# A fused three-stage kernel on one core: the fifth pass of the up projection as two 64-row matmuls, chunks in pairs

## The reference

```python
# x: (2, 4096, 192); weight: 8 heads x 7 taps, each head has 24 of the 192 channels
out = np.einsum('hk,bskhg->bshg', w, x_unf)          # a causal mix of 7 tokens, w = softmax(weight)
h = x @ w_in                                          # 8192 x 192 @ 192 x 2048
g = np.where(h >= 1, h, np.where(h <= -1, 0.0, (h + 1) ** 2 / 4))
x = g @ w_out                                         # 8192 x 2048 @ 2048 x 192
h = x @ w_in2
r = np.maximum(h, 0.0)
g = s * (r * r) + b
return g @ w_out2
```

## Time and profile before

| what | value |
|---|---|
| median of 3 runs | 1198.95 us |
| span of the profiled execution (first to last instruction) | 1196.3 us |
| PE busy | 1177.9 us, 98% of the span, 5138 matmuls |
| PEld busy | 963.1 us, 81%, 5138 loads |
| DVE busy | 934.8 us, 78% |
| ACT busy | 614.1 us, 51% |
| DMA | 20.31 MB, mean 17 GB/s |

### The profile page before, as it was taken

How to read it: one execution, slowest core, us unless ns; L and a number is a source line. 1 busy time by engine, 2 the same in 40 slices (tenths; PEclk the granted TensorE clock), 3 DMA queues, 4 the chain that set the end, 5 groups by cost and what they waited for, 6 DMA issues and landing times.

```text
span 1196.3 us, 14126 instructions
## 1 busy us (share of the span) xinstructions
PE 1177.9 (98%) x5138; PEld 963.1 (81%) x5138; DVE 934.8 (78%) x842; ACT 614.1 (51%) x619; POOL 3.4 (0%) x16
## 2 busy tenths in 40 slices
PE   6999999999999999999999999999999999999998
PEld 3787888888888888888888888888888888888886
DVE  8999987778786877868778687787787878765555
ACT  5446654555545554545545554555545455454544
POOL 1000000000000000000000000000000000000000
PEclk9999999999999999999999999999999999999999
DMA  6003100000000000000000000001000000000000
GB/s 176 1 1 97 53 1 1 27 27 1 0 0 27 26 0 0 0 27 26 0 0 0 27 26 0 0 0 53 0 0 0 0 26 0 0 1 1 27 0 27
DMA packets 12360, 20.31 MB, mean 17 GB/s; under 512 B 1072, under 2 KB 5168, under 8 KB 12336
## 3 DMA queue, kind: packets, MB, share of 16 engines
q1 hardware_dynamic: 12256, 19.99, 5.9%
q0 software_dynamic: 64, 0.00, 0.0%
q10 hardware_dynamic: 16, 0.00, 0.0%
HBM read 13.70 MB, written 6.29 MB: 17 GB/s over the span
## 4 chain that ended last, share of the span: by engine, by line
PE 93%; DVE 5%; issue 1%; DMA 0%; SPq 0%; ACT 0%; DVEq 0%; ACTq 0%
PE h L653 46%; PE acc L666 28%; PE acc_rem L675 19%; DVE g L437 1%; DVE g_lo L455 1%; DVE mixed L489 1%; DVE mixed L503 0%; DVE mixed_rem L503 0%; DMA xraw_rem<-in_x 0%; DVE x_rem L516 0%; DVE up_lo L536 0%; DVE up_rem_lo L536 0%; DVE dn_lo L536 0%; DVE g L445 0%; DVE dn_rem L536 0%
## 5 line engine op out<-in xcount | busy, mean ns | idle before, releaser
L439 DVE SCALAR_TENSOR_TENSOR g<-r,scale,h 128x1024 f32<-128x1024 f32 x128 | 163.9, 1280 | 155.2 <-ACT r L287 154.4
L285 ACT ACTIVATE r<-h,half 128x1024 f32<-128x1024 f32 x128 | 143.1, 1118 | 272.0 <-PE h L653 264.8
L287 ACT ACTIVATE r<-h 128x1024 f32<-128x1024 f32 x128 | 131.7, 1029 | 284.9 <-PE h L653 284.3
L437 DVE TENSOR_TENSOR g<-h,r 128x1024 f32<-128x1024 f32 x128 | 156.6, 1223 | 93.3 <-ACT r L285 92.7
L458 DVE SCALAR_TENSOR_TENSOR g_lo<-g,shift,g_hi 128x1024 fp32r<-128x1024 f32 x128 | 163.7, 1279 | 0.0
L666 PE MATMUL acc<-g_hi,dn_hi 128*128 128x512 f32 x512 | 160.0, 394 | 3.1 <-DVE g_lo L455 1.6
L653 PE MATMUL h<-x_hi,up_hi 128*128 128x512 f32 x512 | 157.9, 390 | 3.0 <-DVE g L437 1.7
L653 PE MATMUL h<-x_rem,up_rem_hi 128*128 128x512 f32 x512 | 157.9, 390 | 2.5 <-DVE x_rem L516 2.5
L675 PE MATMUL acc_rem<-g_lo,dn_rem 128*128 128x512 f32 x512 | 157.9, 389 | 0.0
L675 PE MATMUL acc_rem<-g_hi,dn_rem 128*128 128x512 f32 x512 | 157.9, 389 | 0.0
L666 PE MATMUL acc<-g_lo,dn_hi 128*128 128x512 f32 x512 | 157.9, 390 | 0.0
(11 more groups left out here) (87 smaller groups left out, 963.3 us busy)
## 6 DMA issues: line engine op xcount, KB each, us to landing
xraw<-in_x SPq DMA_DIRECT2D x7, 518.0 KB, 4.4
out<-res SPq DMA_DIRECT2D x7, 512.0 KB, 3.3
stage<-in_moe_w_out SPq DMA_DIRECT2D x6, 384.0 KB, 3.4
xraw_rem<-in_x SPq DMA_DIRECT2D x14, 129.5 KB, 4.0
out<-res_rem SPq DMA_DIRECT2D x7, 256.0 KB, 3.6
stage<-in_moe_w_in SPq DMA_DIRECT2D x2, 512.0 KB, 5.2
stage<-in_moe_w_in SPq DMA_DIRECT2D x4, 256.0 KB, 5.2
xraw<-in_x SPq DMA_DIRECT2D x1, 512.0 KB, 4.2
```

Source lines behind the costliest of these rows:

```text
L285: nc.scalar.activation(r[k][:], h[k][:], ACT.Relu, scale=0.5, bias=half[:, 0:1]).then_inc(r_ready, 1)
L287: nc.scalar.activation(r[k][:], h[k][:], ACT.Relu).then_inc(r_ready, 1)
L437: nc.vector.tensor_tensor(g[k][:], h[k][:], r[k][:], ALU.max).then_inc(h_used, 1)
L439: nc.vector.scalar_tensor_tensor(g[k][:], r[k][:], scale[:, 0:1], h[k][:], ALU.mult, ALU.mult).then_inc(h_used, 1)
```

## The change

The fifth pass is made of 64-row matmuls: batch 0 uses rows 0 to 63 of the array and batch 1 rows 64 to 127 (`up_halves`), each reading only the half of `x_rem` with the high part. The product of the low weights with the low data, which the 128-row form added in, is no longer computed. For this the output of layer 0 must have its high half at rows 64t as the mixed data do: `y_rem` becomes its own tile of 128 x 512, and the ACT and DVE steps that write and split it become two of 64 x 512 each, where they were one of 64 x 1024.

`up` is replaced by `up_pair`: four full passes of chunk j, its two halves, the two halves of chunk j+1, and then the four full passes of chunk j+1. After it come down(j-2) and down(j-1). ACT and DVE follow: the rounding and the low part of chunk j-1 for even j now stand ahead of relu(j) and first(j). In DVE's layer 0 the second step of an odd chunk stands behind the low part of the even one, as before.

```diff
@@ -82,7 +82,7 @@
         mixed_rem = sb("mixed_rem", [P, T])
         shared = sb("shared", [P, B, T])
         fold = shared[0:REM]
-        y_rem = shared[REM:P]
+        y_rem = sb("y_rem", [P, T])
         y = sb("y", [P, B, T])
         res = sb("res", [P, B, T])
         res_rem = sb("res_rem", [REM, B, T])
@@ -141,6 +141,7 @@
         acc_drained = sem("acc_drained")
         fold_ready = sem("fold_ready")
         rem_drained = sem("rem_drained")
+        y_rem_ready = sem("y_rem_ready")
         main_summed = sem("main_summed")
         rem_summed = sem("rem_summed")
         half_drained = sem("half_drained")
@@ -337,11 +338,13 @@
                     act.wait_ge(h_ready, S_free + 1)
                 nc.scalar.activation(dst[0][:], y[:], ACT.Copy).then_inc(x_hi_done[1], 1)
 
-            def round_y_rem(phase, dst, S_free):
-                act.wait_ge(rem_drained, phase + 1)
-                if S_free is not None:
-                    act.wait_ge(h_ready, S_free + 1)
-                nc.scalar.activation(dst[2][REM:P], y_rem, ACT.Copy).then_inc(x_rem_hi_done[1], 1)
+            def round_y_rem(blk, dst, S_free):
+                for t in range(B):
+                    act.wait_ge(y_rem_ready, 2 * blk + t + 1)
+                    if S_free is not None:
+                        act.wait_ge(h_ready, S_free + 1)
+                    rows = slice(t * REM, (t + 1) * REM)
+                    nc.scalar.activation(dst[2][rows, t, :], y_rem[rows], ACT.Copy).then_inc(x_rem_hi_done[1], 1)
 
             def weights_hi(layer, n):
                 kind, q = PIECES[n]
@@ -356,14 +359,16 @@
 
 
                 for j in range(CH):
+                    if j == 0:
+                        if before is not None:
+                            round_g(before, S0 - 1, 1, G0)
+                    elif j % 2 == 0:
+                        round_g(layer, S0 + j - 1, (j - 1) % 2, G0 + j)
                     relu(layer, S0 + j, j % 2)
                     if j == CH - 1:
                         for f in last or ():
                             f()
-                    if j == 0:
-                        if before is not None:
-                            round_g(before, S0 - 1, 1, G0)
-                    else:
+                    if j % 2:
                         round_g(layer, S0 + j - 1, (j - 1) % 2, G0 + j)
                     if j == 1 and before is not None:
                         drain(before, S0, P0 - 1, blk_before)
@@ -407,12 +412,12 @@
                     12: [lambda: round_mixed(c + 2, X1, S0 - 1)]})
                 phase(0, 1, S1, P1, (c + 2) * CH, blk_before=c, extras={
                     4: [lambda: round_y(P0 - 1, X2, S1 - 1)],
-                    8: [lambda: round_y_rem(P0 - 1, X2, S1 - 1)]})
+                    8: [lambda: round_y_rem(c + 1, X2, S1 - 1)]})
 
             S0, P0 = (LOOPS + 1) * 2 * CH, (LOOPS + 1) * 2
             phase(1, 0, S0, P0, NB * CH, blk_before=NB - 1, extras={
                 4: [lambda: round_y(P0 - 1, X1, S0 - 1)],
-                8: [lambda: round_y_rem(P0 - 1, X1, S0 - 1)]})
+                8: [lambda: round_y_rem(NB - 1, X1, S0 - 1)]})
             phase(1, 1, S0 + CH, P0 + 1, NB * CH, blk_before=NB - 2)
             round_g(1, S0 + 2 * CH - 1, 1, None)
 
@@ -463,12 +468,17 @@
                 dve.wait_ge(fold_ready, phase + 1)
                 if layer == 0:
                     if not (isinstance(blk, int) and blk == 0):
-                        dve.wait_ge(x_rem_lo_done[1], blk)
-                    dst = y_rem
+                        dve.wait_ge(x_rem_lo_done[1], 2 * blk)
+                    nc.vector.tensor_tensor(y_rem[0:REM], acc_rem[0:REM, 0, :], fold[:, 0, :],
+                                            ALU.add).then_inc(y_rem_ready, 1)
+                    dve.wait_ge(y_rem_ready, 2 * blk + 1)
+                    nc.vector.tensor_tensor(y_rem[REM:P], acc_rem[0:REM, 1, :], fold[:, 1, :],
+                                            ALU.add).then_inc(y_rem_ready, 1)
+                    dve.wait_ge(y_rem_ready, 2 * blk + 2)
+                    dve.sem_inc(rem_drained, 1)
                 else:
                     dve.wait_ge(stored, 32 * (blk + 1))
-                    dst = res_rem[:]
-                nc.vector.tensor_tensor(dst, acc_rem[0:REM], fold, ALU.add).then_inc(rem_drained, 1)
+                    nc.vector.tensor_tensor(res_rem[:], acc_rem[0:REM], fold, ALU.add).then_inc(rem_drained, 1)
 
             def mix(blk, part, k):
 
@@ -523,9 +533,11 @@
                                         ALU.subtract).then_inc(x_lo_done[1], 1)
 
             def low_y_rem(blk, dst):
-                dve.wait_ge(x_rem_hi_done[1], blk + 1)
-                nc.vector.tensor_tensor(dst[2][0:REM], y_rem, dst[2][REM:P].bitcast(F32),
-                                        ALU.subtract).then_inc(x_rem_lo_done[1], 1)
+                for t in range(B):
+                    dve.wait_ge(x_rem_hi_done[1], 2 * blk + t + 1)
+                    rows, other = slice(t * REM, (t + 1) * REM), slice((1 - t) * REM, (2 - t) * REM)
+                    nc.vector.tensor_tensor(dst[2][other, t, :], y_rem[rows], dst[2][rows, t, :].bitcast(F32),
+                                            ALU.subtract).then_inc(x_rem_lo_done[1], 1)
 
             def weights_lo(layer, n):
 
@@ -539,18 +551,21 @@
             def phase(layer, before, S0, P0, blk_before=None, extras=None, last=None):
 
                 for j in range(CH):
+                    if j == 0:
+                        if before is not None:
+                            low(before, S0 - 1, 1)
+                    elif j % 2 == 0:
+                        low(layer, S0 + j - 1, 1)
                     first(layer, S0 + j, j % 2)
                     if j == CH - 1:
                         for f in last or ():
                             f()
-                    if j > 0:
-                        low(layer, S0 + j - 1, (j - 1) % 2)
-                    elif before is not None:
-                        low(before, S0 - 1, 1)
+                    if j % 2:
+                        low(layer, S0 + j - 1, 0)
+                    if layer == 0:
+                        second(S0 + j, j % 2)
                     if j == 1 and before is not None:
                         drain_rem(before, P0 - 1, blk_before)
-                    if layer == 0:
-                        second(S0 + j, j % 2)
                     for f in (extras or {}).get(j, ()):
                         f()
 
@@ -636,23 +651,41 @@
 
         @block.tensor
         def _(pe):
-            def up(layer, j, S, xs, split=None):
-
-
-                if not (isinstance(S, int) and S < 2):
-                    pe.wait_ge(h_used, S - 1)
+            def up_wide(layer, j, xs, start, split=None):
+
                 cols = slice(j * P, (j + 1) * P)
                 hi, lo, rem = xs
                 passes = [(up_hi[layer], hi, "hi"), (up_lo[layer], hi, None), (up_hi[layer], lo, "lo"),
-                          (up_rem_hi[layer], rem, "rem"), (up_rem_lo[layer], rem, None)]
+                          (up_rem_hi[layer], rem, "rem")]
                 for n, (w, v, part) in enumerate(passes):
                     if split and part:
                         for done, count in split[part]:
                             pe.wait_ge(done, count)
                     for t in range(B):
                         last = nc.tensor.matmul(h[j % 2][:, t, :], w[:, cols], v[:, t, :],
-                                                start=(n == 0), stop=(n == len(passes) - 1))
-                last.then_inc(h_ready, 1)
+                                                start=(start and n == 0), stop=(not start and n == 3))
+                return last
+
+            def up_halves(layer, j, xs, start):
+
+                cols = slice(j * P, (j + 1) * P)
+                for t in range(B):
+                    rows = slice(t * REM, (t + 1) * REM)
+                    last = nc.tensor.matmul(h[j % 2][:, t, :], up_rem_lo[layer][rows, cols], xs[2][rows, t, :],
+                                            start=start, stop=not start)
+                return last
+
+            def up_pair(layer, j, S, xs, split=None):
+
+
+                if not (isinstance(S, int) and S < 2):
+                    pe.wait_ge(h_used, S - 1)
+                up_wide(layer, j, xs, True, split)
+                up_halves(layer, j, xs, False).then_inc(h_ready, 1)
+                if not (isinstance(S, int) and S < 2):
+                    pe.wait_ge(h_used, S)
+                up_halves(layer, j + 1, xs, True)
+                up_wide(layer, j + 1, xs, False).then_inc(h_ready, 1)
 
             def down(layer, j, S, P0, final=False):
 
@@ -681,14 +714,15 @@
 
             def phase(layer, before, S0, P0, xs, split, weights=None):
 
-                for j in range(CH):
+                for j in range(0, CH, 2):
                     if weights and j in weights:
                         pe.wait_ge(w1_lo_done, weights[j])
```

(13 more changed lines are left out.)

## The result

The changed kernel takes 1191.69 us (median of 4 runs, 1191.32 to 1195.77), the kernel before 1199.09 (4 runs). The ratio is 0.9946 with a 95% interval of 0.9931 to 0.9961: 0.5% faster, 7.4 us by the medians. 1183.5 had been forecast, with 15.6 us of gain.

What follows compares the result with a forecast made beforehand. PE's matmul steps were taken to bound the kernel. From the 1196.3 us span, - 13.9 - 3.4 + 2.8 - 1.0 gave 1180.8, and 1183.5 us with the 2.65 us between span and median; range 1150 to 1222.

Steps and rivals of the forecast that it cites:

- group of halves: PE's fifth pass per pair: four halves with two division changes take 0.798 us in place of 0.907, -13.9 us for 128.
- drained sums: Each phase's first down no longer stops for ACT's copy of the sums: 13 x 0.26 = -3.4 us.
- start: Phase 0: DVE has 7.3 us more than PE, two downs hide 4.5, so PE loses +2.8 us.
- end: Last chunks: two downs cover the relu, round, low chain; the 1.46 us stop shrinks to about 0.5, -1.0 us.
- The bound: PE's matmul steps of 0.227 us set the time, one for one, until DVE becomes late.
- The halves: Four 64-row matmuls take 0.454 + 0.112 = 0.566 us, the second half starting one load behind the first.
- The changes: Each change of the array's division costs PE the restart alone, 0.116 us, between bounds of 0 and 0.28.
- emptying: Rival: at each change PE waits 0.16 us for the last matmul, then pays the 0.116 restart; 1211 to 1225 us, chance 0.20.
- Drain and overlap: By the skill's pages, halves start some 4 ns apart and each change drains 0.16 us: group 0.454 + 0.32 = 0.78 us.
- the drain case: Rival: drain but no restart at each change, group 0.78 to 0.89, 1181 to 1195 us; upper part, 1190 to 1199, chance 0.15.
- The rest rows: Splitting DVE's and ACT's rest-row steps adds 2.4 us on DVE and some 0.2 us a block on ACT, beside PE: nothing.
- DVE's cover: Layer 0 loop phases: DVE waits 8.8 us a phase for ACT's rounding, but 68.1 us fits in PE's 71.7: costs nothing.

Runs made afterwards that it cites:

- e2: Order of before on all engines, with the two 64-row halves in each chunk, so 512 division changes in place of 256: 1245.29 us, ratio 1.0388 to the kernel before.
- e3: Changed kernel with each half matmul issued twice, eight halves between the two changes of a pair: 1250.11 us, ratio 1.0427 to the kernel before.
- e4: Changed kernel with both batches' halves on rows 0 to 63 of the array: 1252.56 us, ratio 1.0447 to the kernel before.
- e6: Changed kernel with the odd chunk's halves moved to the end of its up, four division changes a pair in place of two: 1242.60 us, ratio 1.0367 to before.
- e10: Changed kernel with full 128-row fifth passes plus two extra 64-row matmuls of 8 columns a pair, between two division changes: 1245.34 us, ratio 1.0390 to before.
- e0_after_again: The changed kernel unedited, run again beside the experiments: 1192.24 us, ratio 0.9944 to the kernel before; its profiled span is 1189.9 us.
- e8: Kernel before with only PE's order put in pairs; full fifth passes, ACT, DVE and rest rows as before: 1192.72 us, ratio 0.9952.
- e1: Changed kernel with the fifth pass again as full 128-row matmuls, new order and rest rows kept: 1193.11 us, ratio 0.9955 to the kernel before.
- e5: Changed kernel without the fifth pass at all, so no 64-row matmuls and no division changes: 1092.84 us, ratio 0.9115 to the kernel before.

## Why the prediction was right or wrong

The direction was right and the time lies in the range, but the gain is 7.4 us where 15.6 were forecast, and it has another source. By the spans at full clock, 1196.3 before and 1189.9 after:

| term | forecast | measured |
|---|---|---|
| group of halves, 128 pairs | -13.9 | -1.4 |
| drained sums | -3.4 | -4.0 |
| start | +2.8 | +0.3 |
| end | -1.0 | -1.3 |
| sum | -15.5 | -6.4 |

The group's error of 12.5 us is more than the whole miss; the errors of the order, 3.4 us together, went the other way. That the kernel came out clearly faster is in part luck: of the largest term a tenth came, and the order, that was to bring 1.6 us, brought 5.0.

*The bound.* Right for the loop: PE stops there only for the drained sums before and not at all after, and steps and changes that `e2`, `e3`, `e4`, `e6` and `e10` added came through in every phase between the marks. In phase 0 they mostly did not, since DVE sets the time there.

*The halves.* "The second half starts one load behind the first" was wrong, and to the good: the halves overlap, 0.45 to 0.48 us for four (`e3`), where the sum had 0.566. The step that failed is taking the load interval of the earlier trace rows, two loads for the same rows, for loads to different rows. These start together.

*The changes.* This is the step that sank the forecast: "I take the restart alone, 0.116 us", with the emptying of the array put at nothing. A change costs 0.21 us between the marks by `e6`, `e10` and `e2` (0.197 to 0.204 by the totals), and in the group itself (0.894 - 0.454) / 2 = 0.22, or 0.205 with 0.484 for the halves. The rows split it into 0.09 us in which nothing starts, the restart of 0.116, and some hundredths in the matmuls behind. The 0.09 is what I had argued away with "nothing in it shows an array that had to empty": the stop of the earlier trace rows was no change of division, so it could not show it. The nearest row was near in form, not in kind. The slow steps behind a restart stood in the trace of before and I read only the first. Its timeline went on so:

```profile
178.60 0.62 PE L666 MATMUL acc<-g_hi,dn_lo 128*128 128x512 f32 x2
179.07 0.62 PE L675 MATMUL acc_rem<-g_hi,dn_rem 128*128 128x512 f32 x2
179.52 0.62 PE L675 MATMUL acc_rem<-g_lo,dn_rem 128*128 128x512 f32 x2
```

178.14, 178.60, 179.07: steps of 0.46 and 0.47 in place of 0.454. The sum of the group was 0.798 us and it measured 0.890 to 0.900, so that this term gave 0.9 to 1.4 us of its 13.9. The two errors, some 0.1 us too much for the halves and 2 x 0.1 too little for the changes, go opposite ways.

*Drain and overlap.* The Trainium skill, "TensorEngine Tiling (Array Packing)", section "Tiling Modes", says that a change of mode drains the engine. The trace agrees that one must wait, with 0.09 us rather than the 0.16 by which I had priced that drain, and `e10` shows the wait with 8 columns as with 512. The Trainium skill, "TensorE: Matmul & The Clock Gate", section "Part 3", has matmuls on different row tiles start some 4 ns apart; the windows above agree, to their 0.01 us. Drain and overlap by those pages, 0.78 us a group, were nearer on the halves than my own value, but like it they left out the restart.

*The rivals.* None of the cases is the one that came. There is a wait (0.09 us, where emptying had been priced at 0.16) and a restart, and the halves overlap: group 0.454 + 0.44, next to the break-even point at 0.907. With full overlap that point is 0.227 us a change, and 0.22 was paid. The time of 1191.7 lies in the upper part of the drain case, which had 0.15, but the order's gain brought it there and not that mechanism.

*The drained sums.* Right: -3.4 forecast, 4.0 measured by the marks (0.29 a phase; the slow steps behind each restart are the rest), and the waits are gone.

*The start.* +2.8 forecast, +0.3 measured at the first mark. The stop at the end of phase 0 did grow, 0.64 us to 2.03 (`e0_after_again`):

```profile
92.14 0.70 PE L665 MATMUL h<-x_hi,up_hi 128*128 128x512 f32 x2 [2.03 <-DVE g L442]
```

but the first chunks' downs, which before waited 1.08 us for their `g_lo` at us 28.3, now stand behind one more `up` and stop by 0.2 to 0.3. The added wait for `h_used` between the halves, which I had at nothing, stopped PE once, by 0.26 us at us 37. I had priced the loss at the phase's end and not what the same order saves at its beginning.

*The end.* -1.0 forecast, -1.3 measured.

*The rest rows and DVE's cover* cost nothing that shows in the loop, as said: `e8` and `e1`, without and with ACT's and DVE's new lists and rest rows, differ by 0.4 us, which by the marks arises at the start, and `e5` shows the cover holding in the loop with 7 us less of PE in a phase. In phase 1, which the prediction also gave nothing, it held for the changed kernel (72.35 us) and broke in `e5`.

So the title's edit, the two 64-row matmuls, is worth 0.9 us of the 6.6 between `e0_after_again` and before. The pairs, brought in to halve the number of changes, are worth the rest, by what they do at the phase ends, and would have been without any half matmul (`e8`).

What stays open is what the 0.09 us are made of, why a restart is followed by some slow steps, and why four more halves took 0.03 us more than two steps; no run here takes them apart. Making every matmul of the stream 64 rows high, so that no change is left, would have two row groups accumulate into the same sums with nothing to order them. It was not tried.

## What to carry to other kernels

Half-height matmuls on the two halves of the array are worth a step for each pair of them, but entering and leaving that division costs about 0.2 us each: here, with steps of 0.227 us, four halves to a group only break even. More per group would pay, by an estimate: the eight halves of `e3` take 0.894 + 0.484 = 1.38 us with their two changes, where eight full matmuls take 1.81. No kernel here uses it. When an edit needs another order around it, run that order alone: here it carried six sevenths of the gain. And price an event that the trace doesn't show by the nearest row plus what that row can't contain; here the row of a stop could not contain a change of mode.
